# Product and remainder of the quotient for two groups in one VectorE operation, and GpSimd's product held

## The chip, the cores and the metric

The program runs on one core of a Trainium2 chip. The metric is the device time of one execution in microseconds. Five engines work side by side and meet through semaphores: TensorE (PE, matmuls), VectorE (DVE), ScalarE (ACT), GpSimd (POOL) and SyncE (SP, which issues DMAs). SBUF and PSUM are the on-chip memories. Each engine runs its own instructions in the order in which they are written, so a wait holds all that is queued behind it.

## What is computed

Two stages, cut to what matters. A spectral one mixes the channels of each frequency and thresholds the result; a feed-forward one has a quotient of two polynomials as its nonlinearity:

```python
# x: (4, 3008, 256); w_r, w_i: (256, 256)
X = rfft(x, axis=1)
Yr = Xr @ w_r - Xi @ w_i + b_r
Yi = Xr @ w_i + Xi @ w_r + b_i
Yr = sign(Yr) * maximum(abs(Yr) - 0.01, 0)      # Yi in the same way
x = irfft(Yr + 1j * Yi, n=3008, axis=1)         # 12032 tokens of 256

h = x @ w_in                                    # 256 -> 2048
P = a[0] + a[1] * h + a[2] * h**2 + a[3] * h**3
Q = 1.0 + abs(b[0]) * abs(h) + abs(b[1]) * h**2
out = (P / (Q + 1e-6)) @ w_out                  # 2048 -> 256
```

## The kernel before

Tokens go in 26 tiles of 470 (the last has 282), and the 2048 hidden channels of a tile in eight groups of two blocks of 128. That makes 208 groups, and a group is one array of 128 partitions by 940 elements. The main loop of every engine runs over slots q = 0 to 209, eight to a tile, with the engines at different groups:

- TensorE, slot q: `group_f2_hi` (L567, L569) and `group_f2_lo` (L582) of group q-3, which multiply the rounded quotient g_hi and its rest g_lo by w_out. Then `group_f1` (L552) of group q+2 into one of two PSUM buffers h_ps, once VectorE is done with group q there. Behind it come spectral steps where a table has them.
- ScalarE, slot q: den = |h| (L776), sq = h² (L779) and num (L782) of group q+1, each scaled. Then, of group q, the reciprocal of the denominator in two steps in sq (L846, L849).
- GpSimd, slot q: the product g_lo (L1148) of group q-3. Then the DMA that adds sq to den (L1140) for group q+1.
- VectorE, slot q: L1087 and L1090 finish the numerator of group q out of h_ps. `multiplied` (L1067) of group q-2 forms denominator times g_hi. `rounded` (L1062) of group q-1 forms g_hi = (num + a0) / denominator, rounded. `remainder` (L1073) of group q-2 forms (num + a0) minus that product. The rest times the reciprocal is GpSimd's g_lo.

num, sq and den have four buffers, taken by group modulo 4. ScalarE overwrites den once the remainder of the group four before is done (n_rest), and sq once its g_lo is (n_g). g_hi has three buffers, g_lo two.

The spectral steps of batches 1 to 3 run between the groups, up to slot 141. A step c starts in an even slot e: TensorE transforms it (L469). In slot e+1 ScalarE writes xt (L722), VectorE its lower part (`lower_x`, L945, L948), and TensorE the mixing matmuls (L477 to L487). In slot e+2 ScalarE writes neg (L739), between sq and num of its group, and VectorE the soft threshold (`soft`, L954), which reads neg. In slot e+3 TensorE multiplies back (L493) and ScalarE writes it out (L750). Twice a tile, in slots 1 and 3 of its eight, TensorE also makes half of the next tile's input (L529), after that L750; in the slot behind, ScalarE writes yt_hi (L762) ahead of its den, and VectorE yt_lo (`split_lo`, L1022) behind `rounded`.

The order is written out by hand in these loops. Semaphores count finished operations: n_hi for `rounded`, n_back for `multiplied`, n_rest for `remainder`. xw and s1w are the buffers of the first transform's input and output; the last such step is in slot 70.

## Time and profile before

| | us |
|---|---|
| median of 3 runs | 1444.81 |
| lowest and highest | 1444.78, 1445.6 |
| the profiled execution | 1446.29 |
| its span, first to last instruction | 1444.1 |
| TensorE, VectorE busy | 1391.0, 1333.8 |
| ScalarE, GpSimd busy | 1251.6, 632.8 |

Busy time of TensorE is modelled for the ends of its matmuls. For VectorE the start of the next operation is the better measure, since one starts shortly before the other ends. The chain of work that ended last is TensorE for 53% of the span, VectorE for 19% and ScalarE for 16%. A slot is what lies between two starts of L1087; the n-th of them is slot n, counted from 0.

### The profile page before, as it was taken

How to read it: one execution, taken by the hardware profiler on the slowest of the kernel's cores; microseconds unless marked ns; L12 is line 12 of the kernel's file. 1: busy time of each engine (PE TensorE's matmuls, PEld its weight loads, DVE VectorE, ACT ScalarE, POOL GpSimd, SP SyncE). 2: the span in 40 equal slices, each digit the busy share in tenths (PEclk: the TensorE clock that was granted, in tenths of full speed). 3: DMA queues.
4: the chain of work that ended last, by engine and by line, in shares of the span. 5: the costliest groups of instructions: out<-in, count | busy, mean ns of one | idle time of the engine just before them, and what ended most of it. 6: DMA issues, size and time to landing. Idle time of an engine off the chain costs nothing.

```text
span 1444.1 us, 21576 instructions
## 1 busy us (share of the span) xinstructions
PE 1391.0 (96%) x7498; PEld 974.2 (67%) x7498; DVE 1333.8 (92%) x1650; ACT 1251.6 (87%) x1657; POOL 632.8 (44%) x417
## 2 busy tenths in 40 slices
PE   7998999999999999999999999999999999999987
PEld 2776667677666676776767776776766666666666
DVE  5576989989999999999999999999999999999998
ACT  3577989988989889888889989988989999999986
POOL 0000544444445444444445445545445555555554
PEclk8999999999999999999999999999999999999999
DMA  8885666666456656555555555555545555555443
GB/s 260 250 266 142 146 156 138 135 140 150 102 118 154 146 112 140 128 115 122 121 108 127 121 113 118 129 111 111 114 109 108 107 94 112 117 108 110 86 97 70
DMA packets 97913, 188.07 MB, mean 130 GB/s; under 512 B 11216, under 2 KB 57744, under 8 KB 97808
## 3 DMA queue, kind: packets, MB, share of 16 engines
q0 software_dynamic: 29952, 98.58, 36.8%
q1 hardware_dynamic: 67856, 88.12, 20.7%
q8 instruction: 62, 1.02, 0.3%
q14 instruction: 43, 0.35, 0.1%
HBM read 50.60 MB, written 37.49 MB: 61 GB/s over the span
## 4 chain that ended last, share of the span: by engine, by line
PE 53%; DVE 19%; ACT 16%; issue 8%; DMA 2%; POOL 1%; SPq 0%; ACTq 0%; DVEq 0%; POOLq 0%
PE h_ps L552 18%; PE o_ps L582 6%; PE o_ps L567 6%; PE o_ps L569 6%; DVE den L1067 4%; DVE num L1073 4%; DVE num L1087 4%; DVE g_hi L1062 4%; PE d L529 3%; ACT num L782 3%; ACT sq L779 3%; ACT den L776 3%; ACT sq L846 3%; PE d L493 2%; PE o_ps L463 2%
## 5 line engine op out<-in xcount | busy, mean ns | idle before, releaser
L1148 POOL TENSOR_TENSOR g_lo<-num,sq 128x940 fp32r<-128x940 f32 (+1 forms) x205 | 469.5, 2290 | 99.7 <-DVE num L1073 99.5
L1140 POOL DMA_DIRECT2D den<-sq x208 | 182.8, 879 | 698.9 <-ACT sq L779 369.0
L567 PE MATMUL o_ps<-g_hi,wout_hi 128*128 128x470 f32 (+1 forms) x832 | 342.1, 412 | 0.9 <-DVE g_hi L1062 0.9
L569 PE MATMUL o_ps<-g_hi,wout_lo 128*128 128x470 f32 (+1 forms) x832 | 310.5, 374 | 0.0
L552 PE MATMUL h_ps<-yt_hi,win_hi 128*128 128x470 f16 (+1 forms) x832 | 301.9, 363 | 5.3 <-DVE num L1090 5.3
L552 PE MATMUL h_ps<-yt_hi,win_lo 128*128 128x470 f16 (+1 forms) x832 | 300.1, 361 | 0.0
L552 PE MATMUL h_ps<-yt_lo,win_hi 128*128 128x470 f16 (+1 forms) x832 | 300.1, 361 | 0.0
L1087 DVE TENSOR_TENSOR num<-h_ps,num 128x940 f32<-128x940 f32 (+1 forms) x208 | 232.1, 1116 | 33.8 <-ACT num L782 33.0
L1090 DVE SCALAR_TENSOR_TENSOR num<-num,coef,h_ps 128x940 f32<-128x940 f32 (+1 forms) x208 | 245.2, 1179 | 7.4
L1067 DVE SCALAR_TENSOR_TENSOR den<-den,g_hi 128x940 f32<-128x940 f32 (+1 forms) x208 | 244.2, 1174 | 0.1
L1062 DVE SCALAR_TENSOR_TENSOR g_hi<-num,a_sb,sq 128x940 fp32r<-128x940 f32 (+1 forms) x208 | 244.3, 1174 | 0.0
L1073 DVE SCALAR_TENSOR_TENSOR num<-num,a_sb,den 128x940 f32<-128x940 f32 (+1 forms) x208 | 244.2, 1174 | 0.1
L779 ACT ACTIVATE sq<-h_ps,coef 128x940 f32<-128x940 f32 (+1 forms) x208 | 214.8, 1033 | 27.4 <-POOL g_lo L1148 26.2
L582 PE MATMUL o_ps<-g_lo,wout_hi 128*128 128x470 f32 (+1 forms) x832 | 213.8, 379 | 21.8 <-POOL g_lo L1148 21.0
L782 ACT ACTIVATE num<-h_ps,coef 128x940 f32<-128x940 f32 (+1 forms) x208 | 234.5, 1127 | 0.0
L846 ACT ACTIVATE sq<-den,qone 128x940 f32<-128x940 f32 (+1 forms) x208 | 223.8, 1076 | 3.9 <-DMA den<-sq 3.8
L776 ACT ACTIVATE den<-h_ps,coef 128x940 f32<-128x940 f32 (+1 forms) x208 | 213.2, 1025 | 5.8 <-DVE num L1073 4.2
L849 ACT ACTIVATE sq<-sq 128x940 f32<-128x940 f32 (+1 forms) x208 | 203.2, 977 | 6.6
L582 PEld LDWEIGHTS o_ps<-g_lo,wout_hi 128*128 128x128 f32 x832 | 152.2, 189 | 56.5 <-POOL g_lo L1148 37.6
L567 PEld LDWEIGHTS o_ps<-g_hi,wout_hi 128*128 128x128 f32 x832 | 157.9, 190 | 30.9 <-issue 8.3
L569 PEld LDWEIGHTS o_ps<-g_hi,wout_lo 128*128 128x128 f32 x832 | 158.0, 190 | 23.5 <-issue 7.5
L552 PEld LDWEIGHTS h_ps<-yt_hi,win_hi 128*128 128x128 f16 x832 | 81.2, 98 | 115.4 <-issue 47.9
(161 smaller groups left out, 1581.1 us busy)
## 6 DMA issues: line engine op xcount, KB each, us to landing
den<-sq POOLq DMA_DIRECT2D x200, 470.0 KB, 4.4
spec<-s1w SPq DMA_DIRECT2D x64, 192.0 KB, 2.8
z_in<-spec SPq DMA_DIRECT2D x96, 128.0 KB, 2.6
spec<-s_out SPq DMA_DIRECT2D x96, 128.0 KB, 1.9
xw<-in_x SPq DMA_DIRECT2D x31, 384.0 KB, 4.8
out_t<-o_sb SPq DMA_DIRECT2D x25, 470.0 KB, 4.2
zp_in<-spec SPq DMA_DIRECT2D x22, 480.0 KB, 5.4
inv_in<-in_inv SPq DMA_DIRECT2D x96, 64.0 KB, 2.3
```

The lines of the kernel that those rows point to most:

```text
L552: mm = pe.matmul(h_ps[q % 2][:, j, 0:cols(q)], w[:, h, f * P:(f + 1) * P], y[t % 2][:, h, 0:cols(q)], start=i == 0, stop=i == len(terms) - 1)
L567: pe.matmul(o_ps[:, h, 0:w], wout_hi[:, f, h * P:(h + 1) * P], g_hi[q % 3][:, j, 0:w], start=f == 0, stop=False)
L569: mm = pe.matmul(o_ps[:, h, 0:w], wout_lo[:, f, h * P:(h + 1) * P], g_hi[q % 3][:, j, 0:w], start=False, stop=False)
L582: mm = pe.matmul(o_ps[:, h, 0:w], wout_hi[:, f, h * P:(h + 1) * P], g_lo[q % 2][:, j, 0:w], start=False, stop=f == FB - 1)
L779: act.activation(ring(sq, q), h, ACT.Square, scale=scales(q // SLOTS, 3)).then_inc(n_sq, 1)
L782: act.activation(ring(num, q), h, ACT.Identity, bias=scales(q // SLOTS, 4), scale=scales(q // SLOTS, 5)).then_inc(n_num, 1)
L846: act.activation(ring(sq, q), ring(den, q), ACT.Abs_reciprocal_sqrt, bias=qone[:, 0:1]).then_inc(n_rs, 1)
L1062: dve.scalar_tensor_tensor(out=g_hi[r % 3][:, :, 0:w], in0=ring(num, r), scalar=a_sb[:, 0:1], in1=ring(sq, r), op0=ALU.add, op1=ALU.mult). ...
L1067: dve.scalar_tensor_tensor(out=ring(den, r), in0=ring(den, r), scalar=1.0 + 1e-6, in1=g_hi[r % 3][:, :, 0:cols(r)].bitcast(F32), op0=ALU.a ...
L1073: dve.scalar_tensor_tensor(out=ring(num, r), in0=ring(num, r), scalar=a_sb[:, 0:1], in1=ring(den, r), op0=ALU.add, op1=ALU.subtract).then_ ...
L1087: dve.tensor_tensor(top, h, top, ALU.mult).then_inc(n_n2, 1)
L1148: pool.tensor_tensor(g_lo[r % 2][:, :, 0:cols(r)], ring(num, r), ring(sq, r), ALU.mult).then_inc(n_g, 1)
```

## The change

Groups 80 to 197 are taken in 59 pairs (even, odd).

- `multiplied_pair` does the product of both groups of a pair in one operation, at the end of the even slot behind the pair's second `rounded`, behind `soft` too. `remainder_pair` does both remainders in one, in the odd slot that follows, ahead of `rounded`. Each counts one on its semaphore, which `back_steps` converts.
- TensorE's `group_f2_*` and GpSimd's g_lo of a paired group come in slot r+4, where they came in r+3. Slot 83 has none; slot 201 has those of groups 197 and 198.
- GpSimd's g_lo of a paired group waits, besides n_rest, in an even slot for the `rounded` of the slot before, in an odd slot for the merged product of the slot before.
- From group 80 num, den and sq have six buffers. The fifth and sixth lie in xw and s1w. ScalarE waits once, in its first two uses, for these to be free. Its waits ahead of den and sq then look six groups back. g_hi has four buffers, in two pairs.
- In the set-up `pick` is bf16 and `bias_rest` lies in neg.

```diff
@@ tables
+PAIRED = range(80, 198)
 def f2_slot(r):
+    if r in PAIRED:
+        return r + 4
     return r + 3 if late(r) else r + 2
+def back_steps(r):
+    pairs = sum(1 for s in PAIRED if s % 2 == 1 and s < r)
+    return r + 1 - pairs - (r in PAIRED and r % 2 == 1)
+def place(q):
+    return q % 4 if q < PAIRED[0] else (q - PAIRED[0] + 4) % 6
+def user_before(q):
+    if q < PAIRED[0]:
+        return q - 4 if q >= 4 else None
+    return q - 6 if q >= PAIRED[0] + 2 else None
@@ buffers
-        bias_rest, pick = sb("bias_rest", P, D), sb("pick", P, P)
+        pick = sb("pick", P, P, dt=BF16)
...
+        num_pairs, den_pairs = [several(n, 2, P, 2, GB * BANK) for n in ("num", "den")]
+        num_pairs.append(xw[:, 0:2, :, :].rearrange("p i a d -> p i (a d)"))
+        den_pairs.append(xw[:, 2:4, :, :].rearrange("p i a d -> p i (a d)"))
...
+        sq += [s1w[:, 2 * i:2 * i + 2, :].rearrange("p i d -> p (i d)") for i in range(2)]
...
@@ ScalarE, group(q)
-                if q >= 4:
-                    act.wait_ge(n_rest, q - 3)
+                before = user_before(q)
...
+                if before is not None:
+                    act.wait_ge(n_rest, back_steps(before))
                 act.activation(ring(den, q), h, ACT.Abs, scale=scales(q // SLOTS, 2)).then_inc(n_den, 1)
-                if q >= 4:
-                    act.wait_ge(n_g, q - 3)
+                if before is not None:
+                    act.wait_ge(n_g, before + 1)
@@ VectorE
+            def multiplied_pair(r):
+                dve.wait_ge(n_hi, r + 2)
+                dve.scalar_tensor_tensor(out=both(den_pairs, r), in0=both(den_pairs, r), scalar=1.0 + 1e-6,
+                                         in1=g_hi_pairs[r // 2 % 2][:, :, :].bitcast(F32),
+                                         op0=ALU.add, op1=ALU.mult).then_inc(n_back, 1)
+            def remainder_pair(r):
+                dve.wait_ge(n_back, back_steps(r))
+                dve.scalar_tensor_tensor(out=both(num_pairs, r), in0=both(num_pairs, r), scalar=a_sb[:, 0:1],
+                                         in1=both(den_pairs, r), op0=ALU.add, op1=ALU.subtract).then_inc(n_rest, 1)
@@ VectorE, slot q
+                if q - 3 in PAIRED and q % 2 == 1:
+                    remainder_pair(q - 3)
                 if 0 <= q - 1 < NS:
                     rounded(q - 1)
...
+                if q - 2 in PAIRED and q % 2 == 0:
+                    multiplied_pair(q - 2)
@@ GpSimd, slot q
+                for r in [r for r in (q - 4, q - 3, q - 2) if 0 <= r < NS and f2_slot(r) == q and not on_vector(r)]:
+                    pool.wait_ge(n_rest, back_steps(r))
+                    if r in PAIRED and q % 2 == 0:
+                        pool.wait_ge(n_hi, q - 1)
+                    elif r in PAIRED:
+                        pool.wait_ge(n_back, back_steps(q - 3))
```

VectorE in slots 100 and 101, which have a yt_lo and a threshold, and a lower part, before:

```order
L1087 TENSOR_TENSOR num<-h_ps,num 128x940
L1090 SCALAR_TENSOR_TENSOR num<-num,coef,h_ps 128x940
L1067 SCALAR_TENSOR_TENSOR den<-den,g_hi 128x940
L1062 SCALAR_TENSOR_TENSOR g_hi<-num,a_sb,sq 128x940
L1022 SCALAR_TENSOR_TENSOR yt_lo<-d,coef,yt_hi 128x470
L1073 SCALAR_TENSOR_TENSOR num<-num,a_sb,den 128x940
L954 SCALAR_TENSOR_TENSOR ythr,soft_sum<-d,neg 128x256
L1087 TENSOR_TENSOR num<-h_ps,num 128x940
L1090 SCALAR_TENSOR_TENSOR num<-num,coef,h_ps 128x940
L1067 SCALAR_TENSOR_TENSOR den<-den,g_hi 128x940
L945 SCALAR_TENSOR_TENSOR xt<-d,x_scale,xt 128x2x128
L948 TENSOR_SCALAR xt<-xt 128x4x64
L1062 SCALAR_TENSOR_TENSOR g_hi<-num,a_sb,sq 128x940
```

And now; L1138 and L1141 are the former L1087 and L1090, L1102 is `rounded`, L1113 and L1119 are the merged product and remainder, L1062 is yt_lo, L985 and L988 the lower part, L994 the threshold (xw and s1w stand for the fifth and sixth buffers):

```order
L1138 TENSOR_TENSOR num<-h_ps,num 128x940
L1141 SCALAR_TENSOR_TENSOR num<-num,coef,h_ps 128x940
L1102 SCALAR_TENSOR_TENSOR g_hi<-xw,a_sb,s1w 128x940
L1062 SCALAR_TENSOR_TENSOR yt_lo<-d,coef,yt_hi 128x470
L994 SCALAR_TENSOR_TENSOR ythr,soft_sum<-d,neg 128x256
L1113 SCALAR_TENSOR_TENSOR xw<-xw,g_hi 128x2x940
L1138 TENSOR_TENSOR num<-h_ps,num 128x940
L1141 SCALAR_TENSOR_TENSOR num<-num,coef,h_ps 128x940
L985 SCALAR_TENSOR_TENSOR xt<-d,x_scale,xt 128x2x128
L988 TENSOR_SCALAR xt<-xt 128x4x64
L1119 SCALAR_TENSOR_TENSOR xw<-xw,a_sb 128x2x940
L1102 SCALAR_TENSOR_TENSOR g_hi<-num,a_sb,sq 128x940
```

The product has moved from third place to the end, behind the threshold, and the remainder from ahead of the threshold into the next slot, ahead of `rounded`. In slots 162 and 163, which have no spectral step, it reads now:

```order
L1138 TENSOR_TENSOR num<-h_ps,num 128x940
L1141 SCALAR_TENSOR_TENSOR num<-num,coef,h_ps 128x940
L1102 SCALAR_TENSOR_TENSOR g_hi<-num,a_sb,sq 128x940
L1113 SCALAR_TENSOR_TENSOR den<-den,g_hi 128x2x940
L1138 TENSOR_TENSOR num<-h_ps,num 128x940
L1141 SCALAR_TENSOR_TENSOR num<-num,coef,h_ps 128x940
L1119 SCALAR_TENSOR_TENSOR num<-num,a_sb,den 128x2x940
L1102 SCALAR_TENSOR_TENSOR g_hi<-num,a_sb,sq 128x940
L1138 TENSOR_TENSOR xw<-h_ps,xw 128x940
```

Here the merged product follows directly on the `rounded` (L1102) whose g_hi it reads. GpSimd's queue around slot 100, the g_lo of two slots and their DMAs, before:

```order
L1148 TENSOR_TENSOR g_lo<-num,sq 128x940 [waits f2,n_rest]
L1140 DMA den<-sq 128x940 [waits n_sq,n_den]
L1148 TENSOR_TENSOR g_lo<-num,sq 128x940 [waits f2,n_rest]
L1140 DMA den<-sq 128x940 [waits n_sq,n_den]
L1148 TENSOR_TENSOR g_lo<-num,sq 128x940 [waits f2,n_rest]
L1140 DMA den<-sq 128x940 [waits n_sq,n_den]
```

And now, with the additional wait on n_hi or n_back in turn:

```order
L1207 TENSOR_TENSOR g_lo<-xw,s1w 128x940 [waits f2,n_hi,n_rest]
L1195 DMA den<-sq 128x940 [waits n_sq,n_den]
L1207 TENSOR_TENSOR g_lo<-xw,s1w 128x940 [waits f2,n_back,n_rest]
L1195 DMA xw<-s1w 128x940 [waits n_sq,n_den]
L1207 TENSOR_TENSOR g_lo<-num,sq 128x940 [waits f2,n_hi,n_rest]
L1195 DMA xw<-s1w 128x940 [waits n_sq,n_den]
```

What is queued behind each product is the same DMA as before.

## Rows read from the trace of the kernel before

**Rows 1.** The page's first part: busy us, share of the span, instructions.
```profile
PE 1391.0 (96%) x7498; PEld 974.2 (67%) x7498; DVE 1333.8 (92%) x1650; ACT 1251.6 (87%) x1657; POOL 632.8 (44%) x417
```

**Rows 2.** Windows, slots 80-143 and 144-197: us; PE, PEld, DVE, ACT, POOL busy.
```profile
674.87:1086.91 412.04, 402.98 (x2225) 288.57 (x2224) 398.24 (x486) 365.10 (x457) 197.58 (x128) 1.00 0.54 115
1086.91:1389.00 302.09, 294.24 (x1448) 195.50 (x1447) 299.52 (x272) 283.68 (x306) 167.19 (x108) 1.00 0.53 107
```

**Rows 3.** Timeline of VectorE, a late slot: start us, us, line, operation.
```profile
1204.77 1.12 DVE L1087 TENSOR_TENSOR num<-h_ps,num 128x940 f32<-128x940 f32 x1
...
1209.20 1.19 DVE L1073 SCALAR_TENSOR_TENSOR num<-num,a_sb,den 128x940 f32<-128x940 f32 x1
1210.31 1.13 DVE L1087 TENSOR_TENSOR num<-h_ps,num 128x940 f32<-128x940 f32 x1
```

**Rows 4.** Timeline of VectorE, slot 100, to the start of slot 101.
```profile
803.37 1.13 DVE L1087 TENSOR_TENSOR num<-h_ps,num 128x940 f32<-128x940 f32 x1
804.53 1.19 DVE L1090 SCALAR_TENSOR_TENSOR num<-num,coef,h_ps 128x940 f32<-128x940 f32 x1
805.64 1.13 DVE L1067 SCALAR_TENSOR_TENSOR den<-den,g_hi 128x940 f32<-128x940 f32 x1
806.69 1.19 DVE L1062 SCALAR_TENSOR_TENSOR g_hi<-num,a_sb,sq 128x940 fp32r<-128x940 f32 x1
807.80 0.70 DVE L1022 SCALAR_TENSOR_TENSOR yt_lo<-d,coef,yt_hi 128x470 f16<-128x470 f32 x1
...
809.91 0.42 DVE L954 SCALAR_TENSOR_TENSOR ythr<-d,neg 128x256 f32<-128x256 f32 x1 [0.30 <-ACT neg L739]
...
810.93 1.14 DVE L1087 TENSOR_TENSOR num<-h_ps,num 128x940 f32<-128x940 f32 x1 [0.59 <-ACT num L782]
```

**Rows 5.** Waits: us in total, times, longest; two of 675:1087, one of 1135:1385.
```profile
DVE num L1087 <- ACT num L782: 7.3, 13, 0.9
PE o_ps L582 <- POOL g_lo L1148: 5.2, 2, 3.6
...
ACT sq L779 <- POOL g_lo L1148: 10.1, 20, 0.6
```

**Rows 6.** Timelines of GpSimd and VectorE where they overlap, and L1067's mean, 1132:1355.
```profile
1199.12 2.51 POOL L1148 TENSOR_TENSOR g_lo<-num,sq 128x940 fp32r<-128x940 f32 x1
...
1201.31 1.33 DVE L1067 SCALAR_TENSOR_TENSOR den<-den,g_hi 128x940 f32<-128x940 f32 x1
...
1405.71 2.19 POOL L1148 TENSOR_TENSOR g_lo<-num,sq 128x940 fp32r<-128x940 f32 x1 [1.11 <-DVE num L1073]
...
1407.03 1.86 DVE L1067 SCALAR_TENSOR_TENSOR den<-den,g_hi 128x940 f32<-128x940 f32 x1
...
L1067 DVE SCALAR_TENSOR_TENSOR den<-den,g_hi 128x940 f32<-128x940 f32 x40 | 46.5, 1164 | 0.0
```

**Rows 7.** Timelines of VectorE (starts of slots 98, 99, 102) and ScalarE, slots 98 to 102.
```profile
790.68 1.13 DVE L1087 TENSOR_TENSOR num<-h_ps,num 128x940 f32<-128x940 f32 x1
...
795.76 0.22 ACT L739 ACTIVATION_READ_ACCUMULATOR neg<-d,x_lam 128x1 f32 x1
...
797.17 1.13 DVE L1087 TENSOR_TENSOR num<-h_ps,num 128x940 f32<-128x940 f32 x1
...
806.90 0.66 ACT L762 ACTIVATE yt_hi<-d,coef 128x470 f16<-128x470 f32 x1 [1.44 <-PE d L529]
...
809.66 0.22 ACT L739 ACTIVATION_READ_ACCUMULATOR neg<-d,x_lam 128x1 f32 x1
...
817.14 1.13 DVE L1087 TENSOR_TENSOR num<-h_ps,num 128x940 f32<-128x940 f32 x1
...
820.84 0.20 ACT L739 ACTIVATION_READ_ACCUMULATOR neg<-d,x_lam 128x1 f32 x1
```

**Rows 8.** Timeline of TensorE, the products with g_lo of slots 99 and 101.
```profile
799.94 1.02 PE L582 MATMUL o_ps<-g_lo,wout_hi 128*128 128x470 f32 x4
...
813.87 1.01 PE L582 MATMUL o_ps<-g_lo,wout_hi 128*128 128x470 f32 x4
```

More of the change, by code:

```diff
@@ L301, in ring, with both @@
         def ring(tiles, q):
-            return tiles[q % 4][:, 0:GB * cols(q)].rearrange("p (j n) -> p j n", j=GB)
+            return tiles[place(q)][:, 0:GB * cols(q)].rearrange("p (j n) -> p j n", j=GB)
+        def both(pairs, q):
+            return pairs[place(q) // 2][:, :, 0:GB * cols(q)]
         zp_count = []
@@ L653, in _ @@
             for q in range(NS + 2):
-                done = [r for r in (q - 3, q - 2) if 0 <= r < NS and f2_slot(r) == q]
+                done = [r for r in (q - 4, q - 3, q - 2) if 0 <= r < NS and f2_slot(r) == q]
                 for r in done:
@@ L1101, in _ @@
                                               coef[0:ROWS, i, 0:1], None, ALU.mult).then_inc(k_c5, 1)
-                if 0 <= q - 2 < NS and late(q - 2):
+                if 0 <= q - 2 < NS and late(q - 2) and q - 2 not in PAIRED:
                     multiplied(q - 2)
@@ L1113, in _ @@
                     split_lo(S5_AT[q - 1], d0[:, :])
-                if 0 <= q - 2 < NS and late(q - 2):
+                if 0 <= q - 2 < NS and late(q - 2) and q - 2 not in PAIRED:
                     remainder(q - 2)
@@ L1139, in tail @@
                 pool.wait_ge(n_sq, q + 1)
[L1140 removed]
+                pool.dma_start(den[place(q)][:, 0:w], sq[place(q)][:, 0:w], accum_op=ALU.add).then_inc(s_q[q % 4], 16)
             tail(0)
             for q in range(NS + 2):
[L1144 to L1145 removed]
+                for r in [r for r in (q - 4, q - 3, q - 2) if 0 <= r < NS and f2_slot(r) == q and not on_vector(r)]:
[4 more added lines that the diff above has]
+                        pool.wait_ge(n_back, back_steps(q - 3))
                     if r >= 2:
```

35 lines of the change are left out of this document (20 added, 15 removed).

## The prediction

> **What bounds the kernel now.** I call one turn of the eight-per-tile loop a slot and name it by its number in the code; it starts where VectorE starts L1087. The page's first part comes first: TensorE is busy 96% and VectorE 92% of the span, ScalarE 87%, GpSimd 44% [rows 1]. A share of the whole says little here, so the next view is the table of busy times in the two stretches that the change touches [rows 2]. In slots 80 to 143 (674.87 to 1086.91, 412 us, 6.44 us a slot) the spectral steps of the later batches run between the groups, and TensorE, at 403 of 412 us, is as full as VectorE at 398. In slots 144 to 197 (1086.91 to 1389, 5.59 us a slot) they have ended, and VectorE alone is full: 299.5 of 302 us. The rows of single instructions then tell what a slot is made of. In the late stretch it is five VectorE operations back to back, 5.54 us from one L1087 to the next [rows 3]. In the earlier one a slot also carries one of the spectral chain's steps; slot 100, the example below, takes 803.37 to 810.93, 7.56 us [rows 4]. There VectorE waits twice, for ScalarE's neg (0.30 us) and for its num. The table of waits of that stretch says where this sum stays small: 7.3 us for num in 13 places, and TensorE waits 5.2 us for GpSimd's product [rows 5]. So VectorE is the bound late; earlier TensorE and VectorE share it, and a loss on either is felt.
>
> **Merging: what two operations save.** The cost of an operation is the time to the start of the next. For L1067 (a constant as scalar) that is 1.05 us, for L1062 and L1073 (scalar from a tile) 1.11 us [rows 3, 4]. A lane takes an element in 1.04 ns: against the 470 elements of L1022, 0.70 us, an operation of 940 with a tile's scalar takes 1.19 us [rows 4], 0.49 us for 470. So 940 elements are 0.98 us and what is fixed is 0.07 us for L1067 and 0.13 us for L1073. One operation over 1880 elements should cost 2.03 and 2.09 us. A pair of groups saves 0.07 + 0.13 = 0.20 us. It gives some back where the merged product stands straight behind the rounding that it reads: L1087 lasts 1.13 us and the dependent L1090 starts 1.16 us after it [rows 4], 0.03 behind its end, while independent ones start 0.08 before it; that is 0.11 us. So 0.20 us a pair where another step lies between them, 0.09 us where none does.
>
> The skill has a price for this, in a sentence of its own: the Trainium skill (DVE Microarchitecture Reference, "Measured stream behaviour on trn2") puts the fixed part at about 75 ns an instruction; with 118 fewer instructions that would be 8.9 us, near 1436 us, if all of it lay on the path, and it agrees with the row of L1067 and not with that of L1073.
>
> **Late stretch.** Slots 144 to 197 hold 27 pairs, nothing lies between, VectorE is the bound: 27 x 0.09 = -2.4 us.
>
> GpSimd's product slows VectorE where it overlaps an operation with both inputs in SBUF. The product normally starts 0.17 us behind L1087 and lasts 2.2 us, and the next such operation isn't hurt. At 1199.12 it lasted 2.51 us, behind its queue's DMA, and L1067 took 1.33 us where 1.13 is its time [rows 6]. At 1405.71 it overlapped more and L1067 took 1.86 us [rows 6]. Over 40 of the late slots L1067's mean is 1.164 us [rows 6], 0.034 above its 1.13, so the 54 slots have 1.8 us of this in all, and L1087 may add a little: 2 us. The product comes late there because ScalarE's sq, and with it the DMA, waits for the product four groups earlier (10.1 us in 20 places [rows 5]). With six buffers for sq that wait goes, and the product should come on time: -1.5 us, between -2 and 0. The hold itself adds nothing here. The product of slot q waited for an operation at the end of slot q-1, and waits for another one at the same place. What is late next is still VectorE.
>
> The Trainium skill (SBUF — State Buffer, "Who interferes with whom") says that a VectorE instruction with two SBUF inputs and a GpSimd one that reads SBUF exclude each other; by that rule, the 1.86 us row agrees and the hold is right, but it would be worth no more than the 2 us above.
>
> **Slots 80 to 143: the order of the steps is the price.** This is where I expect the loss. In an even slot VectorE now runs L1087, L1090, rounding, yt_lo where there is one, then the soft threshold (L954), and behind it the 2.03 us of the merged product. Before, all five operations stood ahead of the soft threshold. It waits for ScalarE's neg, which was nearly late already. With ScalarE's rows kept, slot 98 (from 790.68): neg ends at 795.98 [rows 7], 5.30 us into the slot, while the threshold is now due at 2.27 + 1.11 + 0.61 = 3.99. The threshold starts 796.01, takes 0.34, the product 2.03: the slot ends at 798.38 where it ended at 797.17 [rows 7], 1.21 us late. Slot 100: neg ends at 809.88, then 0.34 + 2.03 give 812.28 against 810.93 [rows 4, 7], 1.35 us late. In slot 102, without yt_lo, neg ends 3.90 us into the slot (817.14 to 821.04 [rows 7]) and is due at 3.38; starting 1.2 us late against ScalarE, VectorE doesn't wait there.
>
> Late is not lost as long as others have slack. Who waits for that: GpSimd's product of slots 99 and 101 is held until the merged product ends, so it starts 0.17 behind L1087 and ends at 798.38 + 0.17 + 2.20 = 800.75, and at 814.65. TensorE came to its L582 at 799.94 and 813.87 [rows 8]. It waits 0.8 us each time, with the next hidden group (L552) queued behind, and that feeds ScalarE, so the schedule moves as a whole and the two stalls add. Of the 16 such slots in eight tiles 14 have a threshold, and slot 83 has no product (its group comes one slot later): 13 x 0.8 = +10.4 us. Against it, VectorE catches up by 0.20 us a pair, 32 x 0.20 = 6.4 us, but TensorE is nearly full in most slots and takes only part; I let 4 us of it count, 0.5 us a tile: +6.4 us, between +4.0 and +10.4. If GpSimd's freed ScalarE brings neg early enough this term falls to about -1; its waits for the product are short there, so I don't count on it.
>
> **The seam.** In slot 201 groups 197 and 198 both come due, two products stand in GpSimd's queue, 2.2 us each, ahead of a DMA, while VectorE runs its SBUF operations, which there already lose 0.7 us to one product [rows 6]. From 0 to +3 us; I take +1.5, one blocked operation and a half. The waits for xw and s1w to be free cost nothing: the last step that uses them is 10 slots before. The bf16 pick and the bias buffer are set-up work, below 0.1 us.
>
> **Sum.** -2.4 - 1.5 + 6.4 + 1.5 = +4.0 us. The profiled execution has a span of 1444.1 us; 1446.29 us is its time, 1.5 above the median 1444.81 of the runs, to which I add: 1448.8 us.
>
> **Rivals.**
> - Faster: the neg comes early. ScalarE no longer waits for GpSimd's product before sq and may run up to a slot ahead, so the threshold, even in mid slot, finds its neg ready and TensorE its product. For it: the gate on sq is a real row. Against: in slot 100 ScalarE's chain hangs on TensorE's step ahead of yt_hi (1.44 us idle [rows 7]), not on the gate. Then -1 for the early stretch, -2.4 - 2 late, +1 seam: -4.4, 1440.4 us. Chance 0.23, the fixed costs by the skill's figure included.
> - No change: TensorE absorbs most, with half of the 13 stalls: +5.2 - 4 = +1.2, and -2.4 - 1.5 + 1.5: 1443.6 us; or up to 1447.7. Chance 0.25.
> - Much slower: nothing is caught up, all 13 stalls at 0.8 and the seam at 3: +10.4 + 3 - 2.4 = +11, 1455.8 us. It decides from where TensorE has no slack at all. Chance 0.12.
> - That the hold does nothing: in slots without a spectral step it is met at the same moment as the wait before; this is built into the sum.
>
> **Numbers.** The forecast has 0.40. Below 0.2% (2.9 us), about what a measurement of this kernel can tell, a difference is the same. Faster 0.23, same 0.25, slower 0.52. The range from 1440 to 1455 leaves some 0.1 out on each side.
>
> **What would show it.** After: slots 144 to 197 at 5.50 us with merged operations of 2.1 to 2.2 us; ScalarE's wait for the product before sq gone. In slots 80 to 143: VectorE waiting over 15 us in total for neg, TensorE for the product near 10 us, 6.5 us a slot or more. The prediction is wrong if L954's wait stays at some 2 us, or if slots 80 to 143 take less than 412 us, or if a merged operation takes under 2.0 us or well over 2.3.

## The result, and the profile after

The changed kernel takes 1456.85 us (median of 4 runs, 1456.46 to 1457.91), the kernel before 1445.2 us in the same comparison (1444.78 to 1446.97). The ratio is 1.0079, 95% interval 1.0062 to 1.0097. It is slower by 11.65 us where +4.0 was forecast, and 1.85 us above the range. The profiled executions differ by 10.5 us (1456.79 against 1446.29), since the one of before was 1.1 us above that 1445.2. All stretches and waits below come from profiled executions, the times of whole kernels from medians.

The first line of the page after answers to [rows 1]. All engines are as busy as before to within some us, except VectorE, which has 118 fewer operations and 7.4 us less work:

```profile
PE 1390.2 (96%) x7498; PEld 973.3 (67%) x7498; DVE 1326.4 (91%) x1532; ACT 1247.7 (86%) x1657; POOL 635.2 (44%) x417
```

So what was added is idle time, and the two stretches say where. The columns are those of [rows 2]; slots 80 to 143 come first, 144 to 197 second, each from one start of the operation that was L1087 (L1138 now):

```profile
675.08:1097.55 422.47, 402.42 (x2214) 285.48 (x2213) 391.99 (x423) 364.89 (x457) 195.68 (x127) 1.00 0.53 113
1097.55:1397.65 300.10, 293.72 (x1448) 195.81 (x1446) 296.99 (x218) 281.23 (x305) 168.00 (x108) 1.00 0.53 107
```

| Stretch | before | after | difference | forecast |
|---|---|---|---|---|
| to slot 80 | 674.87 | 675.08 | +0.2 | 0 |
| slots 80 to 143 | 412.04 | 422.47 | +10.4 | +6.4 |
| slots 144 to 197 | 302.06 | 300.10 | -2.0 | -3.9 |
| slots 198 to 206 | 41.05 | 42.83 | +1.8 | +1.5 |
| slot 207 starts at | 1430.02 | 1440.48 | +10.5 | +4.0 |

**Slots 80 to 143.** VectorE's busy time fell by 6.2 us there, and the stretch grew by 10.4. TensorE's busy time stayed at 402 us while its stretch grew: it stood still 11 us longer (20.05 us in place of 9.06), which is what its waits for g_lo grew by (16.2 us in place of 5.2). Lines have moved: the soft threshold L954 is L994, `rounded` L1102, the merged product L1113, the merged remainder L1119, single ones L1107 and L1124, GpSimd's product L1207, TensorE's product with g_lo L616, its hidden groups L586. These are three rows of the table of waits (675 to 1095: us in total, times, longest); the last two answer to [rows 5]:

```profile
DVE ythr L994 <- ACT neg L773: 23.1, 16, 1.6
PE o_ps L616 <- POOL g_lo L1207: 16.2, 15, 3.5
...
DVE num L1138 <- ACT num L822: 0.3, 2, 0.2
```

VectorE's waits for neg went from 2.4 us in 8 places to 23.1 in 16, its wait for num from 7.3 us to 0.3: each waits at the first place where it needs ScalarE, and that is now the threshold. TensorE waited in two places before and now waits in 15. Two are the old ones, 1.91 us (slot 89) and 3.49 us (slot 143); the other 13 have 10.8 us, 0.83 each. In slots 98 and 99 VectorE looks like this (timeline: start us, us, line, operation, and in brackets the idle time and its releaser):

```profile
797.11 0.70 DVE L1062 SCALAR_TENSOR_TENSOR yt_lo<-d,coef,yt_hi 128x470 f16<-128x470 f32 x1
799.18 0.42 DVE L994 SCALAR_TENSOR_TENSOR ythr<-d,neg 128x256 f32<-128x256 f32 x1 [1.36 <-ACT neg L773]
...
799.53 2.11 DVE L1113 SCALAR_TENSOR_TENSOR den<-den,g_hi 128x1880 f32<-128x1880 f32 x1
801.55 1.13 DVE L1138 TENSOR_TENSOR xw<-h_ps,xw 128x940 f32<-128x940 f32 x1
```

Slot 98 starts at 793.73 and slot 99 at 801.55: 7.82 us, and 7.70 was worked out ahead. The chain of waits, the list that follows the latest releaser back, in order of time (start us, us, what), shows how this becomes a loop:

```profile
798.69 0.46 ACT neg L773 x2
799.18 0.43 DVE ythr L994 x2
799.61 0.49 DVE den L1113
800.10 1.68 issue
801.78 2.22 POOL g_lo L1207
804.05 1.12 PE o_ps L616 x4
805.17 2.40 PE h_ps L586 x12
...
809.42 1.10 PE d L563 x10
...
813.07 0.46 ACT neg L773 x2
813.56 0.43 DVE ythr L994 x2
```

ScalarE, VectorE, GpSimd, TensorE and ScalarE again, from 799.18 to 813.56. The 1.68 us named issue, in which VectorE ran L1113, is GpSimd standing at its hold. TensorE waited 0.75 us for that product at 804.05, in slot 99, and its hidden groups and L563 behind it moved ScalarE's next neg. In this loop the stall of slot 99 is not made good before the next threshold. VectorE does make up a little in the slots between (slot 102 takes 5.77 us for 5.88), but the next stalls of TensorE come all the same.

**Slots 144 to 197.** A pair of slots of VectorE, the answer to [rows 3]:

```profile
1186.73 1.13 DVE L1138 TENSOR_TENSOR num<-h_ps,num 128x940 f32<-128x940 f32 x1
...
1189.01 1.20 DVE L1102 SCALAR_TENSOR_TENSOR g_hi<-xw,a_sb,s1w 128x940 fp32r<-128x940 f32 x1
1190.24 2.12 DVE L1113 SCALAR_TENSOR_TENSOR xw<-xw,g_hi 128x1880 f32<-128x1880 f32 x1
1192.28 1.13 DVE L1138 TENSOR_TENSOR num<-h_ps,num 128x940 f32<-128x940 f32 x1
...
1194.56 2.17 DVE L1119 SCALAR_TENSOR_TENSOR xw<-xw,a_sb 128x1880 f32<-128x1880 f32 x1
...
1197.75 1.13 DVE L1138 TENSOR_TENSOR num<-h_ps,num 128x940 f32<-128x940 f32 x1
```

1186.73 to 1197.75 is 11.02 us for two slots, 5.51 each where it was 5.54. Where nothing disturbs them, a pair of slots takes 11.01 to 11.03 us after and 11.07 to 11.09 before: 0.06 to 0.07 us a pair. From one start to the next the merged product takes 2.04 us (2.03 was derived from rows of 940 elements) and the merged remainder 2.08 (2.09). The dependent product starts 1.23 us after the rounding that it reads. ScalarE's wait for GpSimd's product ahead of sq is gone from the table of 1135 to 1385, as forecast. GpSimd's product still takes 2.46 us or more in one slot of each tile, and there a merged remainder takes 2.31 us for 2.17.

**The end.** Slot 200 takes 7.55 us where it took 5.50. Timelines of VectorE and GpSimd there:

```profile
1413.17 3.14 DVE L1124 SCALAR_TENSOR_TENSOR num<-num,a_sb,den 128x940 f32<-128x940 f32 x1
...
1412.28 3.03 POOL L1207 TENSOR_TENSOR g_lo<-num,sq 128x940 fp32r<-128x940 f32 x1 [0.37 <-issue]
```

Group 197's product is held on n_back of group 198, which has a single product, in the middle of slot 200 and not at its end. So it is let go beside `rounded` and the remainder of 198, and the remainder takes 3.14 us instead of 1.19.

### The profile page after: what moved, and what is told of

Same layout as the page of the kernel before. It is cut to its first block, busy times and chain, and to the rows that moved or that the text cites. A ratio compares the mean times of both kernels' runs of the same rounds, so it can differ in the third digit from the quotient of the medians.

```text
span 1454.9 us, 21462 instructions
## 1 busy us (share of the span) xinstructions
PE 1390.2 (96%) x7498; PEld 973.3 (67%) x7498; DVE 1326.4 (91%) x1532; ACT 1247.7 (86%) x1657; POOL 635.2 (44%) x417
## 4 chain that ended last, share of the span: by engine, by line
PE 55%; DVE 15%; ACT 15%; issue 8%; POOL 4%; DMA 2%; ACTq 0%; SPq 0%; DVEq 0%; POOLq 0%
PE h_ps L586 19%; PE o_ps L616 7%; PE o_ps L601 6%; PE o_ps L603 6%; POOL g_lo L1207 4%; PE d L563 3%; DVE g_hi L1102 3%; ACT den L816 3%; ACT sq L819 2%; PE d L527 2%; DVE den L1113 2%; ACT num L822 2%; ACT sq L886 2%; DVE num L1119 2%; PE o_ps L497 2%
## 5 line engine op out<-in xcount | busy, mean ns | idle before, releaser
L1207 POOL TENSOR_TENSOR g_lo<-num,sq 128x940 fp32r<-128x940 f32 (+1 forms) x163 | 374.7, 2299 | 132.3 <-issue 96.5
L586 PE MATMUL h_ps<-yt_hi,win_hi 128*128 128x470 f16 (+1 forms) x832 | 301.5, 362 | 7.6 <-DVE num L1141 7.6
L586 PE MATMUL h_ps<-yt_lo,win_hi 128*128 128x470 f16 (+1 forms) x832 | 299.4, 360 | 0.0
L586 PE MATMUL h_ps<-yt_hi,win_lo 128*128 128x470 f16 (+1 forms) x832 | 299.3, 360 | 0.0
L616 PE MATMUL o_ps<-g_lo,wout_hi 128*128 128x470 f32 (+1 forms) x832 | 214.8, 380 | 29.9 <-POOL g_lo L1207 29.1
L1138 DVE TENSOR_TENSOR num<-h_ps,num 128x940 f32<-128x940 f32 (+1 forms) x164 | 183.9, 1121 | 25.8 <-ACT num L822 25.4
L1141 DVE SCALAR_TENSOR_TENSOR num<-num,coef,h_ps 128x940 f32<-128x940 f32 (+1 forms) x164 | 194.2, 1184 | 5.8
L616 PEld LDWEIGHTS o_ps<-g_lo,wout_hi 128*128 128x128 f32 x832 | 151.7, 189 | 69.3 <-POOL g_lo L1207 51.2
L1102 DVE SCALAR_TENSOR_TENSOR g_hi<-num,a_sb,sq 128x940 fp32r<-128x940 f32 (+1 forms) x164 | 194.3, 1185 | 0.0
L822 ACT ACTIVATE num<-h_ps,coef 128x940 f32<-128x940 f32 (+1 forms) x164 | 186.0, 1134 | 0.0
L816 ACT ACTIVATE den<-h_ps,coef 128x940 f32<-128x940 f32 (+1 forms) x164 | 168.9, 1030 | 15.8 <-PE h_ps L586 15.3
L886 ACT ACTIVATE sq<-den,qone 128x940 f32<-128x940 f32 (+1 forms) x164 | 177.5, 1082 | 2.3 <-DMA den<-sq 2.3
L819 ACT ACTIVATE sq<-h_ps,coef 128x940 f32<-128x940 f32 (+1 forms) x164 | 169.6, 1034 | 2.5 <-POOL g_lo L1207 2.5
L586 PEld LDWEIGHTS h_ps<-yt_hi,win_hi 128*128 128x128 f16 x832 | 81.1, 97 | 116.7 <-issue 46.3
L586 PEld LDWEIGHTS h_ps<-yt_hi,win_lo 128*128 128x128 f16 x832 | 81.6, 98 | 81.3 <-issue 0.7
L586 PEld LDWEIGHTS h_ps<-yt_lo,win_hi 128*128 128x128 f16 x832 | 82.0, 99 | 61.4 <-issue 0.6
```

The costliest lines, as they stand in the source:

```text
L586: mm = pe.matmul(h_ps[q % 2][:, j, 0:cols(q)], w[:, h, f * P:(f + 1) * P], y[t % 2][:, h, 0:cols(q)], start=i == 0, stop=i == len(terms) - 1)
L616: mm = pe.matmul(o_ps[:, h, 0:w], wout_hi[:, f, h * P:(h + 1) * P], g_lo[q % 2][:, j, 0:w], start=False, stop=f == FB - 1)
L816: act.activation(ring(den, q), h, ACT.Abs, scale=scales(q // SLOTS, 2)).then_inc(n_den, 1)
L819: act.activation(ring(sq, q), h, ACT.Square, scale=scales(q // SLOTS, 3)).then_inc(n_sq, 1)
L822: act.activation(ring(num, q), h, ACT.Identity, bias=scales(q // SLOTS, 4), scale=scales(q // SLOTS, 5)).then_inc(n_num, 1)
L886: act.activation(ring(sq, q), ring(den, q), ACT.Abs_reciprocal_sqrt, bias=qone[:, 0:1]).then_inc(n_rs, 1)
```

## Experiments

**Theory A**, the prediction's: the merged product stands behind a threshold that waits for ScalarE, so GpSimd's held product and with it TensorE are 0.8 us late 13 times; the rest (merging, seam) is small. **Theory B**: six buffers, the product one slot later, the hold or the collisions on SBUF cost it, and the place of the threshold is incidental. **Rival C** within A: it is the hold that carries the wait to TensorE, or VectorE's lateness itself.

| Run | us | ratio to before, interval | slots 80-143 | 144-197 | 198-206 |
|---|---|---|---|---|---|
| before | 1445.2 | | 412.04 | 302.06 | 41.05 |
| the change | 1456.85 | 1.0079 (1.0062 to 1.0097) | 422.47 | 300.10 | 42.83 |
| e1, merged product first | 1446.06 | 1.0002 (0.9993 to 1.0012) | 413.06 | 300.10 | 42.83 |
| e2, no hold | 1542.61 | 1.0664 (1.0641 to 1.0686) | 495.49 | 316.31 | 42.54 |
| e3, e1 without hold | 1465.7 | 1.0131 (1.0114 to 1.0147) | 422.09 | 314.94 | 42.51 |
| e4, pairs from 144 | 1445.63 | 0.9999 (0.999 to 1.0009) | 412.15 | 299.82 | 42.85 |
| e5, seam held on n_rest | 1456.1 | 1.0068 (1.0051 to 1.0085) | 422.22 | 301.11 | 44.54 |
| e6, six buffers, not merged | 1445.88 | 1.0004 (0.9995 to 1.0013) | 413.67 | 302.52 | 40.82 |
| e8, product let go early | 1490.87 | 1.0312 (1.0298 to 1.0326) | 458.25 | 299.92 | 42.83 |
| e9, late pairs, soft seam | 1446.13 | 1.0 (0.9991 to 1.0009) | 412.10 | 301.13 | 41.81 |
| e10, product ahead of the DMA | 1452.96 | 1.0045 (1.003 to 1.006) | 420.84 | 300.01 | 42.85 |

Each ratio is against the kernel before on the same chip (1445.2 to 1446.18 us).

A stretch is read from one trace, and this sets what a difference can mean. The time to slot 80, where the ten changed kernels run the same instructions, is 672.5 to 675.2 us. Slots 144 to 197, the same in the change, e1, e5, e8 and e10 and but for their first slots in e4 and e9, take 299.8 to 300.1 us in five of these and 301.1 in e5 and e9. TensorE's granted clock tells the two apart. In slot 143 TensorE stands still for over 3 us in all of them, and in all but e4 the clock is lower behind that, longest in e5 and e9: its mean in slots 143 and 144 is 0.61 and 0.79 in e5, 0.59 and 0.82 in e9, 0.86 and 0.83 in the change, 0.82 and 0.88 in the kernel before. So a difference of 1 us in a stretch says nothing without the clock beside it.

### e1: the merged product ahead of the threshold

```diff
                     split_lo(S5_AT[q - 1], d0[:, :])
+                if q - 2 in PAIRED and q % 2 == 0:
+                    multiplied_pair(q - 2)
...
                         measure_x(n, d1[:, D:D + S1N])
-                if q - 2 in PAIRED and q % 2 == 0:
-                    multiplied_pair(q - 2)
```

> The changed kernel with one thing moved: in an even slot the merged product stands ahead of the soft threshold again, so the order is rounding, yt_lo, merged product, threshold. Theory A (the threshold waits for neg with 2 us of work queued behind it, and the late slot end holds GpSimd's product and so TensorE): VectorE's wait for neg falls from 23.1 us to under 5, TensorE's wait for g_lo in slots 80 to 143 from 16.2 us to about 5, that stretch from 422.5 us to 410 to 413, the time from 1456.9 to about 1445. Theory B (the loss comes from the later slot of w_out's groups or from the longer operations themselves): the stretch stays above 420 us and the time above 1454.

Measured: 1446.06 us, and 413.06 us for slots 80 to 143. The wait for neg is gone from the table, and slot 98 on VectorE reads:

```profile
795.77 2.11 DVE L1113 SCALAR_TENSOR_TENSOR den<-den,g_hi 128x1880 f32<-128x1880 f32 x1
797.79 0.42 DVE L994 SCALAR_TENSOR_TENSOR ythr<-d,neg 128x256 f32<-128x256 f32 x1
```

Its waits, in the same stretch, with TensorE's back at two:

```profile
DVE yt_lo L1062 <- ACT yt_hi L796: 9.3, 13, 1.2
...
PE o_ps L616 <- POOL g_lo L1207: 5.0, 2, 3.6
```

Two operations in another order, with every buffer, the later product and the hold kept, give back 10.8 us of the 11.65. That the place of the threshold is the cause is shown; by which path it reaches TensorE is the question of e8 and e10. In the stretch e1 gives back 9.4 us of 10.4. The 1.0 left is in slots 80 to 87 (52.15 us, before 50.84): at the end of slot 83, which has no group of w_out, TensorE waits 1.63 us for ScalarE's s_out, and then the granted clock is at its lower level (0.50) from 703 to 706. The prediction's sum has no term for this start of the pairs. In the changed kernel the clock stays up there.

The run says more. It has 4.5 us less VectorE work in slots 80 to 143 than before (393.8 against 398.2 in the windows) and no stall of the new kind, yet from slot 88 on, past that start, it takes 360.91 us against 361.20. Less work on VectorE bought 0.3 us here. That this is so because TensorE is full is read from the busy times (402 of 413 us); no run varied TensorE's load.

### e4: pairs in slots 144 to 197 only

```diff
-PAIRED = range(80, 198)
+PAIRED = range(144, 198)
```

> The changed kernel with its pairs from group 144 on, not 80, so that slots with spectral steps have the old order. Theory A: slots 80 to 143 take 412 us as before, slots 144 to 197 take 300 us as in the changed kernel, the seam in slot 200 costs its 2 us, the time is 1445 us, the same as before. Theory B (something else that the change brings, as the buffers or the set-up, costs the 10 us): above 1450.

Measured: 1445.63 us. Slots 80 to 143 take 412.15 us, as before; 144 to 197 take 299.82, and the end 42.85. The merging is worth 2.2 us and the seam costs 1.8: nothing is left that can be measured. The early stretch is the whole loss, as e1 says in another way.

### e6: six buffers, single operations

```diff
 def f2_slot(r):
-    if r in PAIRED:
-        return r + 4
     return r + 3 if late(r) else r + 2
...
-    pairs = sum(1 for s in PAIRED if s % 2 == 1 and s < r)
-    return r + 1 - pairs - (r in PAIRED and r % 2 == 1)
+    return r + 1
...
-                if 0 <= q - 2 < NS and late(q - 2) and q - 2 not in PAIRED:
+                if 0 <= q - 2 < NS and late(q - 2):
                     multiplied(q - 2)
...
-                if q - 3 in PAIRED and q % 2 == 1:
-                    remainder_pair(q - 3)
...
-                if 0 <= q - 2 < NS and late(q - 2) and q - 2 not in PAIRED:
+                if 0 <= q - 2 < NS and late(q - 2):
                     remainder(q - 2)
...
-                if q - 2 in PAIRED and q % 2 == 0:
-                    multiplied_pair(q - 2)
...
-                    if r in PAIRED and q % 2 == 0:
-                        pool.wait_ge(n_hi, q - 1)
-                    elif r in PAIRED:
-                        pool.wait_ge(n_back, back_steps(q - 3))
```

> The changed kernel with its six buffers from group 80 on and its four of g_hi, but with the old operations: product and remainder for one group each, in their old places, the groups of w_out in slot r+3, no additional hold. Theory: ScalarE's wait for GpSimd's product ahead of sq (10.1 us in slots 144 to 197 before) goes, and nothing else moves, since VectorE is full in the late stretch and TensorE in the earlier one: slots 80 to 143 in 412 us, 144 to 197 in 302 us, time 1445 us. Rival (the buffers are what pays, as the prediction had it with 1.5 us): 300.5 us in the late stretch and 1443.5.

Measured: 1445.88 us; 413.67, 302.52 and 40.82. ScalarE no longer waits for GpSimd's product before sq, and this brings nothing. The rows put more of the DMA's waits on sq than before (1135 to 1385). The first row is of the kernel before, the two behind it of this one (xw and s1w serve it as fifth and sixth buffer):

```profile
POOL den L1140 <- ACT sq L779: 36.8, 16, 2.8
```

```profile
POOL den L1188 <- ACT sq L816: 29.1, 22, 2.8
POOL xw L1188 <- ACT s1w L816: 16.8, 11, 2.8
```

All waits of that DMA together fell, from 87.9 to 68.2 us, and those of the product for the remainder rose from 24.1 to 45.3 us: where the DMA comes earlier, the product waits for VectorE instead. The late product still lasts 2.45 to 2.54 us in one slot of a tile, in the same slots (148, 156, 164 and on) as before. The timelines say what makes sq late there. This is ScalarE before the change, and GpSimd beside it:

```profile
1148.02 0.97 ACT L839 ACTIVATE o_sb<-o_ps 128x940 f32<-128x940 f32 x1
...
1150.89 0.54 ACT L768 ACTIVATE yt_lo<-d 128x470 f16<-128x470 f32 x1
...
1152.26 1.04 ACT L779 ACTIVATE sq<-h_ps,coef 128x940 f32<-128x940 f32 x1
...
1153.85 0.88 POOL L1140 DMA_DIRECT2D den<-sq  x1 [2.79 <-ACT sq L779]
1154.45 2.51 POOL L1148 TENSOR_TENSOR g_lo<-num,sq 128x940 fp32r<-128x940 f32 x1
```

ScalarE works without a gap: it has o_sb and yt_lo to write ahead of this sq, once a tile, and no gate stands in its way. e6 has the same two there. So the term of -1.5 us was nothing. Against this run, which has the same buffers, merging is worth 302.52 - 300.10 = 2.4 us late. Slots 80 to 143 take 1.6 us more than before, 1.5 of it from slot 132 on, where the clock falls once (0.77 in that slot); the rest of it wasn't explained.

### e2 and e3: without the hold

Both remove the same four lines; e3 does it in the order of e1.

```diff
                     pool.wait_ge(n_rest, back_steps(r))
-                    if r in PAIRED and q % 2 == 0:
-                        pool.wait_ge(n_hi, q - 1)
-                    elif r in PAIRED:
-                        pool.wait_ge(n_back, back_steps(q - 3))
```

> The changed kernel without the additional wait of GpSimd's product on n_hi or n_back; it then waits for n_rest and f2 alone. Theory A says that the late slot end harms only through this hold: TensorE's waits for g_lo in slots 80 to 143 (0.76 us in 13 slots) go, and that stretch loses up to 10 us. Against it works what the hold is for: the product then runs beside VectorE's operations with two SBUF inputs, which cost 0.2 to 1.9 us a slot where they overlapped in the traces so far. In slots 144 to 197, 300.1 us with the hold, that would be 311 us at 0.2 us a slot and 350 us at 0.9. If the two block each other outright the product may just wait for the end of the merged operation by itself, and both stretches stay as they are. I expect the overlap to win: 1465 us, between 1447 and 1500.

> Merged product ahead of the threshold, and no additional hold. It tells whether the hold is needed with the better order too. Theory: yes, since n_rest is met a slot earlier with groups in slot r+4, and the product then starts right behind GpSimd's DMA, in mid slot, beside the merged operations: 1500 us or more, as without the hold alone (1542.6). Rival (the hold matters only because VectorE is late at the threshold): 1446 us.

Measured: 1542.61 us for e2, 86 us above the change and far beyond what was expected; 1465.7 us for e3, 20 us above e1 and below what was expected. Timelines of e2, VectorE and GpSimd:

```profile
817.11 4.79 DVE L1113 SCALAR_TENSOR_TENSOR den<-den,g_hi 128x1880 f32<-128x1880 f32 x1
...
817.42 2.49 POOL L1203 TENSOR_TENSOR g_lo<-num,sq 128x940 fp32r<-128x940 f32 x1
...
1324.94 2.12 DVE L1113 SCALAR_TENSOR_TENSOR den<-den,g_hi 128x1880 f32<-128x1880 f32 x1
...
1325.65 3.49 POOL L1203 TENSOR_TENSOR g_lo<-num,sq 128x940 fp32r<-128x940 f32 x1
```

The first pair costs VectorE 2.7 us, the second nothing, but there GpSimd takes 1.3 us longer. The hold is needed with the later product, in either order. The collisions are not all of e2's loss: the stalls that they bring to TensorE are followed by a lower granted clock (0.94 over slots 80 to 143, 1.00 with the change), and TensorE is busy for 429.6 us there in place of 402.4. How much is the one and how much the other was not taken apart. Most of e2's loss is in slots 80 to 143 (495.49 us), where the late threshold puts the merged product beside the free product; with the threshold last the same slots take 422.09, at a clock of 0.98. Late, both lose 15 to 16 us. Theory B is right that the collision is dear, and wrong that the change pays for it: no merged product in the changed kernel is lengthened, and outside the seam only one merged remainder a tile is, by 0.15 us.

### e5 and e9: the seam

```diff
                         pool.wait_ge(n_hi, q - 1)
+                    elif r in PAIRED and r + 1 not in PAIRED:
+                        pool.wait_ge(n_rest, back_steps(q - 3))
                     elif r in PAIRED:
```

> The changed kernel with the hold of group 197's product, in slot 201, on the remainder of group 198 and not on its product. In the changed kernel the product of group 198 is an ordinary one in mid slot 200, so the hold lets GpSimd go there, and its product and the remainder block each other (L1124 takes 3.14 us in place of 1.19). Theory: slot 200 takes 5.5 us in place of 7.55, the time falls by 2 us to 1455. Rival: the two products of slot 201 are late by as much and TensorE loses the 2 us two slots later; then the time stays.

Measured: 1456.1 us. Slot 200 is back at 5.60 us, with L1124 undisturbed:

```profile
1411.32 1.19 DVE L1124 SCALAR_TENSOR_TENSOR num<-num,a_sb,den 128x940 f32<-128x940 f32 x1
...
1415.79 2.78 DVE L1102 SCALAR_TENSOR_TENSOR g_hi<-xw,a_sb,s1w 128x564 fp32r<-128x564 f32 x1
```

But the product hits the next slots: 201 to 203 take 7.18, 4.75 and 4.77 us where the change has 5.15, 4.33 and 3.58. TensorE stands still for 1.8 us there, and behind it the clock is at 0.50 to 0.55 from 1418 to 1421. The price only moves; the end takes 44.54 us against 42.83. The hold is the mechanism of slot 200, not the whole of the seam.

e9 keeps late pairs, puts the product first, and keeps the later product until group 203, where the groups are shorter:

```diff
-PAIRED = range(80, 198)
+PAIRED = range(144, 198)
+SHIFTED = range(144, 204)
...
-    if r in PAIRED:
+    if r in SHIFTED:
         return r + 4
...
+                if q - 2 in PAIRED and q % 2 == 0:
+                    multiplied_pair(q - 2)
...
-                    elif r in PAIRED:
+                    elif r in PAIRED and r + 1 in PAIRED:
                         pool.wait_ge(n_back, back_steps(q - 3))
+                    elif r in SHIFTED:
+                        pool.wait_ge(n_rest, back_steps(q - 3))
```

> Pairs only from group 144 to 197, the merged product ahead of the threshold, and w_out's groups one slot later from 144 to 203, so that the slot with two of GpSimd's products falls where a group is 564 elements wide. Theory: the late stretch keeps its gain of 2 us (300 us in place of 302), the seam costs 0.5 to 1 us in place of 1.8, the time is 1444.5 us, 0.1% below before at most. Rival: any seam costs its 2 us, then 1445.5.

Measured: 1446.13 us. The end is 1.0 us shorter than with e4. The late stretch is 1.3 us longer, though its instructions are e4's: it goes with the lower clock in slots 143 and 144 and is no price of the edit that can be shown. No version that was run beats the kernel before.

### e8 and e10: does the hold carry the wait?

In slot 98 GpSimd idles while VectorE waits for neg. If the product of slot 99 ran in that gap, TensorE would not see the wait. e8 lets it go earlier, on `rounded` instead of the merged product:

```diff
                     pool.wait_ge(n_rest, back_steps(r))
-                    if r in PAIRED and q % 2 == 0:
+                    if r in PAIRED and (q % 2 == 0 or (q - 3 in S2_AT and q - 2 in S5_AT)):
                         pool.wait_ge(n_hi, q - 1)
```

> The changed kernel with one hold changed: in the odd slots 3 and 5 of a tile whose slot before has a yt_lo and a threshold, GpSimd's product waits for the rounding of the slot before and no longer for its merged product, so that it runs while VectorE waits there for neg. VectorE's own order and its waits stay. Theory A (the wait for neg is passed on to TensorE through the held product): TensorE's wait for g_lo in slots 80 to 143 falls from 16.2 us to some 5, the stretch from 422.5 us to 412 to 414, the time to 1447, although VectorE still waits 20 us or more for neg. Rival C (VectorE's late numerators are what TensorE and ScalarE lack): the stretch stays above 420 us.

Measured: 1490.87 us, a miss. The product still stood behind slot 98's DMA in GpSimd's queue. Timelines of VectorE and GpSimd:

```profile
807.44 4.80 DVE L1113 SCALAR_TENSOR_TENSOR den<-den,g_hi 128x1880 f32<-128x1880 f32 x1
...
807.15 0.86 POOL L1195 DMA_DIRECT2D xw<-s1w  x1 [3.03 <-PE o_ps L616]
807.75 2.50 POOL L1207 TENSOR_TENSOR g_lo<-num,sq 128x940 fp32r<-128x940 f32 x1
```

The gap was full of the DMA's own wait, and the product came out beside the merged product. It says what a collision costs and nothing on the question. The cost has a second part, which TensorE shows in slot 99:

```profile
814.57 0.37 PE L586 MATMUL h_ps<-yt_hi,win_hi 128*128 128x470 f16 x1 [2.52 <-DVE xw L1141]
...
816.28 0.60 PE L586 MATMUL h_ps<-yt_hi,win_hi 128*128 128x470 f16 x1
```

It stood still for 2.52 us, because VectorE freed h_ps late. From 815.2 to 818.6 the granted clock was then at its lower level (0.50), and a matmul started every 0.39 us in place of 0.20. e10 therefore issues the product ahead of that DMA (the body of `product` is the old loop's):

```diff
+            def in_wait(q):
+                return q % 2 == 1 and q - 4 in PAIRED and q - 3 in S2_AT and q - 2 in S5_AT
...
+                    if not in_wait(q):
+                        product(r, q)
+                if in_wait(q + 1):
+                    pool.wait_ge(n_hi, q)
+                    pool.wait_ge(f2, q - 4)
+                    pool.wait_ge(n_rest, back_steps(q - 3))
+                    pool.tensor_tensor(g_lo[(q - 3) % 2][:, :, 0:cols(q - 3)], ring(num, q - 3), ring(sq, q - 3), ALU.mult).then_inc(n_g, 1)
```

> The run before this one left GpSimd's product where its queue has it, behind the DMA that waits for sq, so it didn't run in VectorE's wait but beside the merged product, which it lengthened from 2.11 to 4.80 us. Here the product of the odd slots 3 and 5 of a tile (where the slot before has a yt_lo and a threshold) stands ahead of that DMA in the queue and waits for the rounding of the slot before: it should run from 3.5 to 5.7 us of the even slot, while VectorE waits for neg until 5.4 to 5.8. VectorE's order is that of the changed kernel. Theory A (the wait for neg reaches TensorE through the held product): TensorE's wait for g_lo in slots 80 to 143 falls from 16.2 us to some 6, the stretch from 422.5 us to 412 to 415, the time to 1447 to 1449, with VectorE's wait for neg still near 20 us. Rival C (the late numerators themselves are what the others lack): above 420 us. If the end of the product still overlaps the merged product, some slots take 2.7 us more.

Measured: 1452.96 us, 3.9 us below the change (4.9 by the ratios) and 6.8 above before. Of this gain the traces show 1.6 us in slots 80 to 143 and 1.3 ahead of slot 80, where the two don't differ. The product ran in the gap:

```profile
796.51 2.21 POOL L1219 TENSOR_TENSOR g_lo<-num,sq 128x940 fp32r<-128x940 f32 x1 [1.09 <-DVE g_hi L1102]
```

The 0.75 us stalls at slots 91, 93, 99, 101 and their like are gone. The threshold's wait is as long as it was, and TensorE now waits more for VectorE to free h_ps (675 to 1095):

```profile
DVE ythr L994 <- ACT neg L773: 20.9, 15, 1.6
...
PEld h_ps L586 <- DVE num L1141: 4.9, 9, 2.6
```

In the changed kernel the last row has 2.6 us in one place. Slots 80 to 143 take 420.84 us, 1.6 us less than with the change. So TensorE's wait for g_lo fell as theory A said (16.2 to 7.0 us, some 6 expected), and the stretch did what rival C said (above 420, where A had 412 to 415).

The time from TensorE's first product with g_hi to its first with g_lo, over the 56 slots from 88 on, tells what the hold carried. Summed above its shortest (1.78 to 1.79 us) it is 7.12 us before, 18.76 after, 12.29 here and 6.78 in e1, in stretches of 361.20, 370.53, 367.92 and 360.91 us. With the two products of a tile moved, e10 has 6.5 us of the 11.6 less on this sum, but only 2.6 us of 9.3 less in the stretch. The chain of waits of e10 shows one way that is left, from the threshold of slot 100 on:

```profile
812.28 0.43 DVE ythr L994 x2
812.71 2.03 DVE xw L1113
814.74 1.06 DVE num L1138
...
824.14 2.62 issue
826.77 2.23 POOL g_lo L1205
829.04 1.12 PE o_ps L616 x4
```

VectorE is late behind its wait for neg, runs on without a gap, and the product of slot 103, whose hold the edit left alone, hands this lateness to TensorE. Besides, the clock of e10 is lower in slots 83 and 132 (0.72 and 0.75), and the slots behind them, 84 and 133, take 8.72 and 7.77 us where the change has 7.75 and 6.21. In slot 83 TensorE had waited 2.4 us for h_ps in both kernels, so this may be no effect of the edit. Neither theory A nor rival C is settled by this run: the held products are one way from the threshold to TensorE, VectorE's late start another, and how the remaining 6.7 us divide was not taken apart. Only e1, which takes the wait itself away, closes every way.

## Why the prediction was wrong

The direction was right, and so were the cause (the merged product behind the threshold) and the size of the loss before anything was set against it. What failed is what was set against it: the 4 us of catch-up above all, and the 1.5 us for the product on time. The rival that it called much slower, 1455.8 us and a chance of 0.12, came within 1.1 us. That is in part luck: its sum has the seam at 3 us, which measured 1.8, and leaves out the -1.5 without a reason.

- **What bounds the kernel.** Right for TensorE, wrong in what was made of it. TensorE at 403 of 412 us was called as full as VectorE, and then VectorE was still allowed to catch up.
- **Merging.** Right: 2.04 and 2.08 us measured against 2.03 and 2.09, and -2.0 us against the kernel before, -2.4 against e6, where -2.4 was forecast. An undisturbed pair gained 0.06 to 0.07 us, not 0.09; the rest of the 2.0 us comes from the slots in which a product and VectorE overlap.
- **The product on time, -1.5 us. Failed.** The sq gate was a wait in the table, but not what made the product late: with the gate gone (e6, and the change too) the product still lasts 2.45 us and more in one slot of a tile, since ScalarE has o_sb and yt_lo to write ahead of that sq. A wait that goes is a gain only when nothing else ends at the same time.
- **The threshold in front of the merged product, +10.4 us gross. Right in cause, count and size, right only in part in the path.** 13 new stalls were counted and 13 came, in all 10.8 us. That GpSimd's held product alone carries them to TensorE is not borne out: e10 took nearly all of these stalls away and won 1.6 us of the stretch. Slot 98 is 7.82 us long against 7.70 worked out. Slot 100, worked out by itself from its old start (803.37 to 812.28, 8.91 us), took 8.25: its neg ended 5.85 us into the slot and not 6.51, since VectorE's start of the slot had itself moved.
- **The catch-up, -4 us. Failed, and it is most of the error.** The 0.20 us a pair are real on VectorE (its busy time fell by 6.2 us). They show in its slots too: slot 99 takes 6.13 us for 6.20. But none of this came off TensorE's stalls: ten of the 13 are 0.75 to 0.77 us long, the others 0.78, 1.19 and 1.23, and TensorE stands still 11.0 us longer, as much as its waits for g_lo grew by. e1, with the saving and no stall, is 0.3 us shorter than before from slot 88 on. The stretch grew by 10.4 us, the upper bound that was given: of the 4 us nothing came.
- **The seam, +1.5 us.** Right in size (+1.8), wrong in place and mechanism. It isn't two products in slot 201, but one product let go in mid slot 200 by a count that a single operation reaches sooner than a merged one.
- **Sum.** +10.43 - 1.96 + 1.78 + 0.21 = +10.46 us to the start of slot 207, against +4.0. Of the 6.5 us between, 4.0 are the catch-up and 1.5 the product on time, 0.4 the late stretch (e6, which merges nothing, is 0.5 us longer there than before), 0.3 the seam and 0.2 the slots ahead, less than two traces of the same instructions differ by. The medians differ by 11.65; the remaining 1.1 us are the profiled execution of before, which was 1.1 us above the 1445.2.
- **What would show it.** The waits came as said: 23.1 us for neg (over 15), TensorE 16.2 (near 10 expected), 6.60 us a slot (6.5 or more), the late slots at 5.56 on average (5.50).

The Trainium skill (SBUF — State Buffer, "Who interferes with whom") says that a VectorE instruction with two SBUF inputs and a GpSimd one that reads SBUF exclude each other. The trace agrees: 4.80 us for 2.11 beside a product of 2.50, or 3.49 for 2.2 on the other side. The rule argues for the hold, e2 and e3 bear it out, and it was not what decided this change.

## What to carry to other kernels

When operations are merged or moved, look at what now stands in front of the long one in its queue: an operation that waits for another engine belongs behind the work that others wait for. Here swapping two lines was worth 10.8 us. Credit a saving on one engine against a stall on another only if the other has room; here, with TensorE at 403 of 412 us, nothing came off its 13 new stalls. The reverse doesn't hold: taking the stalls away at TensorE (e10) did not give their time back as long as VectorE still waited. Compare the granted clock of two traces before a difference of 1 us is called a price or a gain. And a hold by a counted semaphore changes its moment where the count goes from merged to single steps.
